# A chunked RWKV recurrence feeding a gated MLP: head pairs two levels apart instead of three, and the weights' low halves made by VectorE

## The chip, the cores and the metric

One Trainium2 chip, one core of it. The metric is device time in microseconds (us) of one execution, as the median of a few runs. Beside it stands one profiled execution, whose trace gives every instruction's start and duration. A core has TensorE (PE in the rows; its weight loads are PEld), VectorE (DVE), ScalarE (ACT), GpSimd (POOL) and SyncE (SP, which only issues DMAs here). The engines run their own instruction lists in order and meet through semaphores.

## What is computed

```python
def _attn_ref(r, k, v, w, u):                # r, k, v, w: [2, 8, 768, 48], u: [8, 48]
    for t in range(S):
        kt, vt, rt, wt = (k[:, :, t], v[:, :, t], r[:, :, t], w[:, :, t])
        cur = np.einsum('bhd,bhe->bhde', u[None] * kt, vt)
        y[:, :, t] = np.einsum('bhd,bhde->bhe', rt, state + cur)
        state = wt[:, :, :, None] * state + np.einsum('bhd,bhe->bhde', kt, vt)

x = y as [2, 768, 384]
h = gelu_tanh(x @ w_in)                      # w_in: [384, 1024]
u, v = h halves; v_n = layernorm(v) * g_ln
v_s = einsum('ts,bsd->btd', w_sg, v_n) + b_sg[None, :, None]
x2 = x + (u * v_s) @ w_out
xk, xr = mixes of x2 and x2 shifted by one token, by mu_k and mu_r
out = sigmoid(xr @ w_r) * (relu(xk @ w_k) ** 2 @ w_v)
```

## The kernel before

**The recurrence.** Two heads form a pair, 8 pairs q = 0 to 7 in all. The sequence of 768 is cut in 12 chunks of 64. Inside a chunk the score matrix with its decays is built in six levels: level 0 gives each token its own block and its partner's, level l joins blocks of 2^l tokens. For each level TensorE multiplies the scaled k by the scaled r (`level_job`, 12 x 2 matmuls), VectorE copies the wanted part into `aT` through a mask (`take_level`), and k and r are then scaled by products of w over blocks of that length: k by VectorE (`scale_k`, tile `kT`), r by VectorE up to level 2 (`scale_r`, tile `r2`) and by GpSimd from level 3 on. GpSimd also makes the products of w (`join`, tiles `wb`, `wchunk`). Level l can start only when both scalings of the level below are done.

**Jobs of a pair.** `w`, `k` and `r` are transposes of the loaded tokens (`turn_job`): TensorE into PSUM banks called `turn`, then ACT copies out (`copy_turn`), and VectorE makes the first scaled half of k and of r (`first_k`, `first_r`) straight from the same banks. The next transpose into these banks waits for both (`turn_free`). `kt` turns the scaled k back, ACT copies it to `ktok`; `u` multiplies it by v to the state increments; VectorE's `chain` scans them; `y` multiplies states and scores into the output, which ACT copies to `yT` and SP stores into `xT`, the transposed x. `sg` transposes one of six row blocks of w_sg, in the `turn` banks too.

**Slots.** The order of all engines comes from a table of slots. Pair q runs level l in slot 3q + l, so two pairs are under way, and there are 30 slots. `pair_jobs` places the other jobs, `SG_SLOTS` the w_sg transposes, `EARLY_DENSE` the first dense groups (the six V and eight U groups of batch 0, in slots 21 to 28), `joins` GpSimd's products.

**The dense part.** All dense matmuls are made exact to fp32 by halves: a = a_high + a_low, and three products of halves (`split`, three matmul lines). ACT casts the high halves of w_in, w_sg and w_out in 15 pieces, one a slot from slot 6 on (`SPLITS`); GpSimd subtracts to get the low halves two slots later (`low_half`). After the last slot TensorE runs the groups in the order G (w_sg), V, O, U, G, K, O, R, P, K, R, P. VectorE's `norm` and `apply_norm` make the layernorm of V of batch 0 in slots 24 and 25, with ACT's square root and casts `high_vn` between them; G needs the result, and w_sg's low halves.

**PSUM.** Eight banks: two `turn`, two for level jobs of even pairs and two of odd ones (`level`), two `ybanks`.

**Loads.** SP issues all DMAs in one list: pair loads wait for the r transpose two pairs back, loads of v for the y job four pairs back, stores of y for ACT's copy.

Of the kernel before, what the change touches and what calls it, by code (L numbers as in the profile page):

```python
# [15 lines left out]
def rwkv_gmlp_channel_mix_kernel(nc, r, k, v, w, u, w_in, g_ln, w_sg, b_sg, w_out,  # L16
# [25 lines left out]
    SLOTS = 3 * NP + LEVELS  # L42
# [7 lines left out]
    def pair_jobs(slot):  # L50

        a = slot // 3
        if slot % 3 == 0:
            jobs = [("kt", a - 2), ("w", a + 1), ("u", a - 2)]
        elif slot % 3 == 1:
            jobs = [("k", a + 1), ("y", a - 2)]
        else:
            jobs = [("r", a + 1)]
        return [(kind, q) for kind, q in jobs if 0 <= q < NP]

    def side_jobs(slot):


        jobs = [("sg", SG_SLOTS.index(slot))] if slot in SG_SLOTS else []
        return pair_jobs(slot) + jobs + EARLY_DENSE.get(slot, [])

    SG_SLOTS = [3, 4, 6, 7, 9, 10]
    EARLY_DENSE = {21: [("V", 0, 0), ("V", 0, 1)], 22: [("V", 0, 2), ("V", 0, 3)], 23: [("V", 0, 4), ("V", 0, 5)],
                   24: [("U", 0, 0), ("U", 0, 1)], 25: [("U", 0, 2), ("U", 0, 3)], 26: [("U", 0, 4), ("U", 0, 5)],
                   27: [("U", 0, 6)], 28: [("U", 0, 7)]}  # L70
# [10 lines left out]
    R_ZEROED, A_ZEROED, VT_ZEROED = (8, 10, 4, 5), (9, 11, 16, 17), 15  # L81
    K_SCALES = [(0, 0)]
    R_SCALES = [(0, 0)]
    for slot in range(SLOTS):
        if slot:
            K_SCALES += [(q, 0) for kind, q in pair_jobs(slot - 1) if kind == "k"]
            R_SCALES += [(q, 0) for kind, q in pair_jobs(slot - 1) if kind == "r"]
        K_SCALES += [(q, l) for q, l in level_jobs(slot) if l]
        R_SCALES += [(q, l) for q, l in level_jobs(slot) if 0 < l < DVE_R]
# [11 lines left out]
    def joins(slot):  # L101

        a, found = slot // 3, []
        for q, l in ([(a, 4), (a, 5), (a + 1, 0)], [(a + 1, 1), (a + 1, 2)], [(a + 1, 3)])[slot % 3]:
            if 0 < q < NP:
                found.append((q, l))
        return found
# [4 lines left out]
    def join_at(q, l):  # L112
        return JOINS.index((q, l)) + 1

    SPLITS = {6: ("in", 0), 7: ("in", 1), 8: ("in", 2), 9: ("in", 3), 10: ("in", 4), 11: ("in", 5),
              12: ("sg", 0), 13: ("sg", 1), 14: ("sg", 2), 15: ("sg", 3), 16: ("sg", 4), 17: ("sg", 5),
              18: ("out", 0), 19: ("out", 1), 20: ("out", 2)}
# [35 lines left out]
    with ExitStack() as ctx:  # L153
# [78 lines left out]
        kT, r2, aT, vt = [None] * 4, [None] * 4, [None] * 4, [None] * 4  # L232
# [9 lines left out]
        assert low[0] >= A_aT, (low[0], A_aT)  # L242
# [42 lines left out]
        level = [ps[:, 2:4, :], ps[:, 4:6, :]]  # L285
        ybanks = ps[:, 6:8, :]
        ybank = [ps[:, 6, :], ps[:, 7, :]]
# [116 lines left out]

        def turn_banks(job):
            kind, q = job
            if job == ("r", 0) or kind == "kt":
                return ybanks
            return level[1] if job == ("k", 0) else turn
# [14 lines left out]
        def _(sp):  # L424
# [76 lines left out]
        def _(pool):  # L501
# [36 lines left out]
            def scale_r(q, l):  # L538
# [6 lines left out]
                t = right2(r2[q % 4][0:ROWS, :, :], h)  # L545
# [3 lines left out]

            def low_half(slot):  # L550
                behind = slot - 2
                if behind in SPLITS:
                    lo, raw, hi = halves(SPLITS[behind])
                    pool.wait_ge(w_high, list(SPLITS).index(behind) + 1)
                    nc.gpsimd.tensor_tensor(lo, raw, hi.bitcast(F32), ALU.subtract).then_inc(w_low, 1)
# [24 lines left out]
            for s in (2, 3):  # L580
                nc.gpsimd.memset(r2[s][:, :, :], 0.0).then_inc(late_zeroed, 1)

            for slot in range(SLOTS):
                for q, l in joins(slot):
                    join(q, l)
# [3 lines left out]
                low_half(slot)  # L589
# [15 lines left out]
        def _(act):  # L605
            def copy_turn(job):
# [4 lines left out]
                if kind == "r":  # L611
                    if q < 4:
# [5 lines left out]
                    for x, (lo, hi) in enumerate(HEADS):  # L618
                        ins = nc.scalar.copy(by_parity(in_banks(r2[q % 4][lo:hi, x, :]))[:, 0],  # L619
# [131 lines left out]
            for slot in range(SLOTS):  # L751
# [14 lines left out]
                if slot == 18:  # L766
                    for m in range(MT):
                        high_x(0, m)
                if slot == 24:
                    root(0)  # L770
                if slot == 25:
# [39 lines left out]
        def _(dve):  # L811
# [20 lines left out]
            def first_r(q):  # L832
# [3 lines left out]
                for x, (lo, hi) in enumerate(HEADS):  # L836
                    ins = nc.vector.tensor_tensor(by_parity(in_banks(r2[q % 4][lo:hi, x, :]))[:, 1],
# [14 lines left out]
            def scale_r(q, l):  # L852
                h = 1 << l
                dve.wait_ge(r_scaled_dve, r_at(q, l - 1))
                t = right2(r2[q % 4][0:ROWS, :, :], h)
# [4 lines left out]
            def take_level(q, l):  # L860
                h = 1 << l
                dve.wait_ge(scores, level_at(q, l) + 1)
                if l == 0:
                    if q < 4:
                        dve.wait_ge(zeroed, A_ZEROED[q])
                    if q == 0:
# [4 lines left out]
                        level[q % 2][:, :, 0:HF].rearrange("p b (m t) -> p b m t", t=CH))  # L871
                else:
                    dve.wait_ge(masked, level_at(q, l - 1) + 1)
                    if q == 0:
# [5 lines left out]
                        level[q % 2][:, l % 2, 0:HF].rearrange("p (m n h) -> p m n h", m=2 * C, h=h))  # L880
                ins.then_inc(masked, 1)

            def chain(q):
# [6 lines left out]
                else:  # L890
# [8 lines left out]
                    in1=ybanks[0:ROWS, 1, 0:D], op0=ALU.mult, op1=ALU.add).then_inc(states, 1)  # L899

# [114 lines left out]
            for slot in range(SLOTS):  # L1015
                for kind, q in pair_jobs(slot - 1) if slot else []:
                    if kind == "k":
                        first_k(q)
                    elif kind == "r":
                        first_r(q)  # L1020
# [5 lines left out]
                for q, l in level_jobs(slot):  # L1026
# [4 lines left out]
                for kind, q in pair_jobs(slot):  # L1031
                    if kind == "u":
                        chain(q)
                if slot == 18:
                    for m in range(MT):
                        low_x(0, m)
                if slot == 19:
# [3 lines left out]
                if slot == 24:  # L1041
                    norm(0)
                if slot == 25:
# [23 lines left out]
        def _(pe):  # L1067
# [46 lines left out]
            def y_job(q):  # L1114
# [3 lines left out]
                for n in range(1, NCH):  # L1118
                    for x, (lo, hi) in enumerate(((0, 64), (64, ROWS))):
                        state = sc_last[0:ROWS, 0:hi - lo] if n == NCH - 1 else sc[0:ROWS, 0:hi - lo, n - 1]  # L1120
                        nc.tensor.matmul(ybanks[lo:hi, n % 2, n // 2 * CH:(n // 2 + 1) * CH], state,  # L1121
                                         r2[q % 4][0:ROWS, x, n * CH:(n + 1) * CH], start=(n < 3), stop=False,
# [9 lines left out]
            def level_job(q, l):  # L1132
                h = 1 << l
                if l == 0:
                    pe.wait_ge(copied, turn_at[("r", q)] + 1)
                    if q == 1:
                        pe.wait_ge(k_scaled, k_at(0, 0))
                    if q >= 2:
                        pe.wait_ge(masked, level_at(q - 2, LEVELS - 1) + 1)
                else:  # L1140
# [5 lines left out]
                    pe.wait_ge(masked, level_at(q, max(l - 2, 0)) + 1)  # L1146
                for c in range(C):
                    for g in range(2):
                        s = slice(c * P + g * CH, c * P + (g + 1) * CH)
                        if l == 0:  # L1150
                            ins = nc.tensor.matmul(  # L1151
                                level[q % 2][CHUNK[g], c // 3, c % 3 * P:(c % 3 + 1) * P].rearrange("p (x t) -> p x t", x=2),
                                kU[0:ROWS, s], rU[0:ROWS, :, s], start=True, stop=True)
                        else:
                            ins = nc.tensor.matmul(  # L1155
                                level[q % 2][CHUNK[g], l % 2, c * CH:(c + 1) * CH].rearrange("p (x t) -> p x t", x=2),
                                kT[q % 4][0:ROWS, s], right2(r2[q % 4][0:ROWS, :, s], h), start=True, stop=True)
# [79 lines left out]
            for slot in range(SLOTS):  # L1237
                for q, l in level_jobs(slot):
                    level_job(q, l)
# [40 lines left out]
```

## Time and profile before

| what | us |
| --- | --- |
| median of 3 runs | 449.48 |
| lowest and highest | 448.78, 451.25 |
| the profiled execution, device time | 453.91 |
| its span, first to last instruction | 452.2 |
| TensorE busy | 390.1 |
| VectorE busy | 259.6 |
| ScalarE busy | 182.5 |
| GpSimd busy | 145.1 |

The span is what the trace shows. The profiled execution took 1.7 us more than its span and 4.4 us more than the median. Times inside the trace are counted from the span's start. A row of a timeline gives start, duration, engine, line and operation, what it writes and reads, how many instructions were merged, and in brackets how long the engine had stood idle and what released it; "issue" there means that the profile names no releaser.

### The profile page before, as it was taken

The numbers are of one execution on the slowest core, as the hardware profiler recorded it, in microseconds if no ns is written. First come the engines' busy times: TensorE is split into PE (matmuls) and PEld (weight loads), VectorE is DVE, ScalarE is ACT, GpSimd is POOL, SyncE is SP. The second block draws the span as 40 slices with busy tenths as digits, with TensorE's granted clock in tenths as the row PEclk, the third lists the DMA queues.
The fourth block names the chain that finished last, engine by engine and source line by source line (L and its number), as shares of the span: only waits on it lengthen the run. The fifth ranks groups of instructions, "written<-read, shape, count | busy, mean of one in ns | idle before, by whom it ended". The sixth has DMA issues, their size and how long they took to land.

```text
span 452.2 us, 9083 instructions
## 1 busy us (share of the span) xinstructions
PE 390.1 (86%) x3836; PEld 367.9 (81%) x3836; DVE 259.6 (57%) x369; ACT 182.5 (40%) x318; POOL 145.1 (32%) x153
## 2 busy tenths in 40 slices
PE   3767687867676679988699999999999999999997
PEld 2656577757666568877599989999999999999997
DVE  6735575768596972667326543599879601565001
ACT  4332554454455233245332140662686630265100
POOL 7624253748393931331000000052195000084000
PEclk9955896988798857999599999999999999999999
DMA  8996423241420100101010000030500001100011
GB/s 157 255 268 194 80 57 77 48 87 39 95 55 2 28 1 1 28 2 28 1 28 1 1 0 1 0 141 0 191 4 1 0 19 52 36 0 1 0 54 52
DMA packets 58584, 23.59 MB, mean 52 GB/s; under 512 B 52656, under 2 KB 56112, under 8 KB 58544
## 3 DMA queue, kind: packets, MB, share of 16 engines
q1 hardware_dynamic: 58544, 23.02, 20.2%
q8 instruction: 30, 0.49, 0.5%
q14 instruction: 10, 0.08, 0.1%
HBM read 18.29 MB, written 2.36 MB: 46 GB/s over the span
## 4 chain that ended last, share of the span: by engine, by line
PE 79%; issue 8%; DVE 7%; ACT 4%; DMA 1%; SPq 1%; ACTq 0%; DVEq 0%
PE ps L1164 18%; PE ps L1165 18%; PE ps L1166 18%; PE ps L1155 7%; PE ps L1151 5%; DVE kT L849 4%; PE ps L1121 3%; PE ps L1088 3%; PE ps L1110 3%; PE ps L1093 2%; PE ps L1098 1%; ACT ktok L641 1%; PE ps L1126 1%; ACT r L619 1%; DVE vn_l L942 1%
## 5 line engine op out<-in xcount | busy, mean ns | idle before, releaser
L1155 PE MATMUL ps<-r,kT 112*64 112x64 f32 x960 | 40.8, 249 | 29.4 <-issue 21.7
L1155 PEld LDWEIGHTS ps<-r,kT 112*64 112x64 f32 x960 | 37.0, 161 | 35.2 <-issue 25.9
L849 DVE TENSOR_TENSOR kT<-kT,wb 112x384 f32<-112x384 f32 x40 | 41.0, 1032 | 30.5 <-PE ps L1155 29.2
L601 POOL TENSOR_TENSOR sq_f<-sq_f 128x384 f32<-128x384 f32 x32 | 33.7, 1071 | 74.9 <-ACT sq_f L734 74.8
L546 POOL TENSOR_TENSOR r<-r,wb 112x768 f32<-112x768 f32 x24 | 39.9, 1663 | 50.8 <-PE ps L1155 50.8
L1010 DVE TENSOR_TENSOR ot<-ps,ee 128x384 f32<-128x384 f32 x12 | 6.7, 558 | 54.6 <-PE ps L1166 54.6
L995 DVE TENSOR_TENSOR sq_l<-sq_f,sq_h 128x384 fp32r<-128x384 f32 x32 | 27.7, 864 | 10.3 <-ACT sq_h L739 10.3
L1166 PE MATMUL ps<-xk_h,wk_l 128*128 128x384 f32 x96 | 32.2, 335 | 0.0
L1165 PE MATMUL ps<-xk_l,wk_h 128*128 128x384 f32 x96 | 32.2, 335 | 0.0
L1164 PE MATMUL ps<-xk_h,wk_h 128*128 128x384 f32 x96 | 32.2, 335 | 0.0
L1164 PE MATMUL ps<-wv_h,sq_h 128*128 128x384 f32 x96 | 32.1, 334 | 0.0
L1166 PE MATMUL ps<-wv_h,sq_l 128*128 128x384 f32 x96 | 32.1, 334 | 0.0
L1165 PE MATMUL ps<-wv_l,sq_h 128*128 128x384 f32 x96 | 32.1, 334 | 0.0
L1164 PE MATMUL ps<-wsg_h,vn_h 128*128 128x384 f32 x96 | 32.1, 334 | 0.0
L1165 PE MATMUL ps<-wsg_l,vn_h 128*128 128x384 f32 x96 | 32.1, 334 | 0.0
L1166 PE MATMUL ps<-wsg_h,vn_l 128*128 128x384 f32 x96 | 32.1, 334 | 0.0
L596 POOL TENSOR_TENSOR wk_l<-wk_raw,wk_h 128x1024 fp32r<-128x1024 f32 x3 | 8.2, 2778 | 65.1 <-ACT wk_h L797 65.1
L1151 PE MATMUL ps<-rU,kU 112*64 112x128 f32 x192 | 22.4, 421 | 7.2 <-ACT r L619 7.2
L1151 PEld LDWEIGHTS ps<-rU,kU 112*64 112x64 f32 x192 | 19.8, 228 | 8.0 <-ACT r L619 8.0
L893 DVE TENSOR_TENSOR_SCAN sc<-wm,ps 112x480 f32<-112x480 f32 x8 | 9.2, 1154 | 27.4 <-PE ps L1110 27.4
L876 DVE COPY_PREDICATED aT<-mask,ps 128x384 f32<-128x384 int8 x40 | 24.8, 656 | 0.2
L856 DVE TENSOR_TENSOR r<-r,wb 112x768 f32<-112x768 f32 x16 | 24.9, 1558 | 0.0
(150 smaller groups left out, 994.6 us busy)
## 6 DMA issues: line engine op xcount, KB each, us to landing
tok_w<-in_w_dram SPq DMA_DIRECT2D x16, 144.0 KB, 3.0
tok_k<-in_k_dram SPq DMA_DIRECT2D x16, 144.0 KB, 3.3
tok_r<-in_r_dram SPq DMA_DIRECT2D x16, 144.0 KB, 3.1
vt<-in_v_dram SPq DMA_DIRECT2D x16, 144.0 KB, 3.3
sgn<-in_moe_w_sg_dram SPq DMA_DIRECT2D x6, 384.0 KB, 5.1
out_dram<-ot SPq DMA_DIRECT2D x12, 192.0 KB, 1.9
xT<-yT SPq DMA_DIRECT2D x12, 144.0 KB, 2.7
win_raw<-in_moe_w_in_dram SPq DMA_DIRECT2D x1, 1536.0 KB, 9.1
```

The costliest lines, as they stand in the source:

```text
L546: nc.gpsimd.tensor_tensor(t, t, pair_of(h, 0, q).unsqueeze(1).unsqueeze(3).broadcast_to([ROWS, 2, S // (2 * h), h]), ALU.mult).then_inc(r_ ...
L601: nc.gpsimd.tensor_tensor(t, t, t, ALU.mult).then_inc(k_sq, 1)
L849: nc.vector.tensor_tensor(t, t, pair_of(h, 1, q).unsqueeze(2).broadcast_to([ROWS, S // (2 * h), h]), ALU.mult).then_inc(k_scaled, 1)
L856: nc.vector.tensor_tensor(t, t, pair_of(h, 0, q).unsqueeze(1).unsqueeze(3).broadcast_to([ROWS, 2, S // (2 * h), h]), ALU.mult).then_inc(r_ ...
L876: ins = nc.vector.copy_predicated(right(aT[q % 4][:, :, :, :].rearrange("p c x t -> p (c x t)"), h), mask[:, l - 1, 0:CH // 2].unsqueeze(1 ...
L995: nc.vector.tensor_tensor(sq_l[:, f, c], sq_f[:, f, c], sq_h[:, f, c].bitcast(F32), ALU.subtract).then_inc(k_low, 1)
L1088: ins = nc.tensor.transpose(dst[0:ROWS, c // 3, c % 3 * P:(c % 3 + 1) * P], tok[q % 2][kind][:, c, :], ident[:, :])
L1151: ins = nc.tensor.matmul(level[q % 2][CHUNK[g], c // 3, c % 3 * P:(c % 3 + 1) * P].rearrange("p (x t) -> p x t", x=2), kU[0:ROWS, s], rU[0 ...
L1155: ins = nc.tensor.matmul(level[q % 2][CHUNK[g], l % 2, c * CH:(c + 1) * CH].rearrange("p (x t) -> p x t", x=2), kT[q % 4][0:ROWS, s], righ ...
L1164: nc.tensor.matmul(acc, ah, bh, start=(i == 0), stop=False)
L1165: nc.tensor.matmul(acc, ah, bl, start=False, stop=False)
L1166: ins = nc.tensor.matmul(acc, al, bh, start=False, stop=(i == n - 1))
```

## The change

Pairs now run two levels apart: pair q has level l in slot 2q + l, three pairs are under way, and there are 22 slots. One table, `pe_jobs`, now gives TensorE's order with the levels placed between the other jobs; ACT follows its side jobs. The two banks of level 0 and 1 are shared by all pairs (`young`), levels 2 and 3 have one bank (`middle`), levels 4 and 5 another (`old`). There is a fifth `r2` buffer. VectorE takes each level right behind its scalings, pair by pair, and makes the 15 low halves, in slots 3 to 8 (w_in), 14 to 19 (w_sg) and 20, 20, 21 (w_out). ACT's casts of the high halves start in slot 2. GpSimd scales r ahead of its joins. The w_sg transposes go to slots 3, 5, 7, 9, 11 and 13, the V groups to slots 16 to 18, the U groups to 19 to 21. SP loads w_in ahead of pair 3, spreads the w_sg loads, asks for pairs earlier, and loads the bias after the last store of y.

```diff
-    SLOTS = 3 * NP + LEVELS
+    SLOTS = 2 * NP + LEVELS
...
-        return [(q, slot - 3 * q) for q in (slot // 3 - 1, slot // 3) if 0 <= q < NP and 0 <= slot - 3 * q < LEVELS]
+        return [(q, slot - 2 * q) for q in (slot // 2 - 2, slot // 2 - 1, slot // 2)
+                if 0 <= q < NP and 0 <= slot - 2 * q < LEVELS]
...
+    def pe_jobs(slot):
+
+        a = slot // 2
+        if slot % 2 == 0:
+            jobs = [("kt", a - 3), ("level", a - 2, 4), ("level", a - 1, 2), ("w", a + 1), ("level", a, 0), ("u", a - 3),
+                    ("k", a + 1)]
         else:
-            jobs = [("r", a + 1)]
-        return [(kind, q) for kind, q in jobs if 0 <= q < NP]
+            jobs = [("level", a - 2, 5), ("level", a - 1, 3), ("r", a + 1), ("level", a, 1), ("y", a - 3)]
+        jobs = [job for job in jobs if 0 <= job[1] < NP]
+        jobs += [("sg", SG_SLOTS.index(slot))] if slot in SG_SLOTS else []
+        return jobs + EARLY_DENSE.get(slot, [])
...
-    SG_SLOTS = [3, 4, 6, 7, 9, 10]
+    SG_SLOTS = [3, 5, 7, 9, 11, 13]
+    EARLY_DENSE = {16: [("V", 0, 0), ("V", 0, 1)], 17: [("V", 0, 2), ("V", 0, 3)], 18: [("V", 0, 4), ("V", 0, 5)],
+                   19: [("U", 0, 0), ("U", 0, 1), ("U", 0, 2)], 20: [("U", 0, 3), ("U", 0, 4), ("U", 0, 5)],
+                   21: [("U", 0, 6), ("U", 0, 7)]}
...
+        return [(q, slot - 2 * q + 1) for q in range(1, NP) if 0 <= slot - 2 * q + 1 < LEVELS]
...
+    SPLITS = {2: ("in", 0), 3: ("in", 1), 4: ("in", 2), 5: ("in", 3), 6: ("in", 4), 7: ("in", 5),
+              8: ("sg", 0), 9: ("sg", 1), 10: ("sg", 2), 11: ("sg", 3), 12: ("sg", 4), 13: ("sg", 5),
+              14: ("out", 0), 15: ("out", 1), 16: ("out", 2)}
+    LOW_SLOTS = [3, 4, 5, 6, 7, 8, 14, 15, 16, 17, 18, 19, 20, 20, 21]
...
-        level = [ps[:, 2:4, :], ps[:, 4:6, :]]
+        young, middle, old = ps[:, 2:4, :], ps[:, 4, :], ps[:, 5, :]
...
             load_pair(2)
+            sp.dma_start(win_raw[:, :, :], w_in.rearrange("(m p) f -> p m f", p=P)).then_inc(win_in, 16)
+            load_pair(3)
+            load_sg(0)
+            load_sg(1)
             load_v(0)
-            for t in range(C):
+            load_pair(4)
+            for t in range(2, C):
                 load_sg(t)
             load_v(1)
-            load_pair(3)
-            sp.dma_start(win_raw[:, :, :], w_in.rearrange("(m p) f -> p m f", p=P)).then_inc(win_in, 16)
+            load_pair(5)
...
-            sp.dma_start(bbc[:, :], b_sg.rearrange("(a s) -> a s", a=1).broadcast_to([P, S])).then_inc(bias_in, 16)
             for q in range(NP):
-                if q + 4 < NP:
-                    load_pair(q + 4)
                 store_y(q)
                 if q + 4 < NP:
                     load_v(q + 4)
+                if q + 6 < NP:
+                    load_pair(q + 6)
+            sp.wait_ge(turned, turn_at[("r", 6)] + 1)
+            sp.dma_start(bbc[:, :], b_sg.rearrange("(a s) -> a s", a=1).broadcast_to([P, S])).then_inc(bias_in, 16)
...
             for slot in range(SLOTS):
-                for q, l in joins(slot):
-                    join(q, l)
                 for q, l in level_jobs(slot):
                     if l >= DVE_R:
                         scale_r(q, l)
-                low_half(slot)
+                for q, l in joins(slot):
+                    join(q, l)
...
                     if 0 < l < DVE_R:
                         scale_r(q, l)
-                for q, l in level_jobs(slot):
                     take_level(q, l)
...
+                for n in range(PIECES):
+                    if LOW_SLOTS[n] == slot:
+                        low_half(n)
...
-                    if q == 1:
-                        pe.wait_ge(k_scaled, k_at(0, 0))
-                    if q >= 2:
-                        pe.wait_ge(masked, level_at(q - 2, LEVELS - 1) + 1)
+                    if q:
+                        pe.wait_ge(masked, level_at(q - 1, 1) + 1)
...
-                    pe.wait_ge(masked, level_at(q, max(l - 2, 0)) + 1)
+                    if l % 2:
+                        pe.wait_ge(masked, level_at(q, l - 1) + 1)
+                    elif q:
+                        pe.wait_ge(masked, level_at(q - 1, l + 1) + 1)
```

What this makes of the order is shown at two places. In these lists `ident` with a `tok` tile is a token transpose, with `kT` the kt job, with `sgn` a w_sg transpose; `rU,kU` is a level 0, `r2...,kT...` a later level, `vt,ktok` the u job (44 matmuls, left out behind the first), `sc` the beginning of a y job.

TensorE, around the period of one pair in the steady part, before:

```order
L1098 MATMUL ps<-ident_58,sgn_79 128x128 x6
L1155 MATMUL ps<-r22_93,kT2_94 64x64 x12
L1155 MATMUL ps<-r23_89,kT3_90 64x64 x12
L1088 MATMUL ps<-ident_58,tok_r0_110 112x128 x6
L1155 MATMUL ps<-r23_89,kT3_90 64x64 x12
L1151 MATMUL ps<-rU_105,kU_104 64x128 x12
L1093 MATMUL ps<-ident_58,kT2_94 128x112 x6
L1088 MATMUL ps<-ident_58,tok_w1_108 112x128 x6
L1110 MATMUL ps<-vt2_91,ktok_83 64x48
```

TensorE, from one w_sg transpose to the y job of the next slot, after:

```order
L1104 MATMUL ps<-ident_58,sgn_79 128x128 x6
L1099 MATMUL ps<-ident_58,kT2_95 128x112 x6
L1162 MATMUL ps<-r23_90,kT3_91 64x64 x12
L1162 MATMUL ps<-r24_87,kT0_103 64x64 x12
L1094 MATMUL ps<-ident_58,tok_w0_112 112x128 x6
L1158 MATMUL ps<-rU_106,kU_105 64x128 x12
L1116 MATMUL ps<-vt2_92,ktok_83 64x48
...
L1094 MATMUL ps<-ident_58,tok_k0_110 112x128 x6
L1162 MATMUL ps<-r23_90,kT3_91 64x64 x12
L1162 MATMUL ps<-r24_87,kT0_103 64x64 x12
L1094 MATMUL ps<-ident_58,tok_r0_111 112x128 x6
L1162 MATMUL ps<-r20_102,kT1_99 64x64 x12
L1127 MATMUL ps<-r22_94,sc_80 64x64
```

The kt job and the u job had one transpose between them and now have two levels, a transpose and a level 0; the w_sg transpose now follows a y job and stands ahead of kt and of both levels of the next slot.

VectorE, one odd slot and what follows it, before (levels of two pairs, scalings of both ahead of the copies):

```order
L828 TENSOR_TENSOR kT0_102<-ps,wT_103 112x384
L849 TENSOR_TENSOR kT2_94<-kT2_94,wb0_84 112x12x32
L849 TENSOR_TENSOR kT3_90<-kT3_90,wb1_85 112x96x4
L856 TENSOR_TENSOR r23_89<-r23_89,wb1_85 112x192x4
L876 COPY_PREDICATED aT2_92<-mask_76,ps 128x12x32
L876 COPY_PREDICATED aT3_88<-mask_76,ps 128x96x4
L837 TENSOR_TENSOR r20_101<-ps,wT_103 48x384 x2
```

VectorE, odd slot 7 and the head of slot 8, after:

```order
L827 TENSOR_TENSOR kT0_103<-ps,wT_104 112x384
L848 TENSOR_TENSOR kT1_99<-kT1_99,wb1_85 112x12x32
L875 COPY_PREDICATED aT1_97<-mask_76,ps 128x12x32
L848 TENSOR_TENSOR kT2_95<-kT2_95,wb0_84 112x48x8
L875 COPY_PREDICATED aT2_93<-mask_76,ps 128x48x8
L848 TENSOR_TENSOR kT3_91<-kT3_91,wb1_85 112x192x2
L855 TENSOR_TENSOR r23_90<-r23_90,wb1_85 112x384x2
L875 COPY_PREDICATED aT3_89<-mask_76,ps 128x192x2
L903 TENSOR_TENSOR win_l_50<-win_raw_51,win_h_49 128x512
L836 TENSOR_TENSOR r24_87<-ps,wT_104 48x384 x2
```

Between first k and the next first r there were five operations and are now eight, the last of them a low half.

## Rows read from the trace of the kernel before

**Rows 1.** The page: the span, and the clock granted to TensorE by slice.

```profile
span 452.2 us, 9083 instructions
...
PEclk9955896988798857999599999999999999999999
```

**Rows 2.** One steady stretch: length, each engine's busy time, granted clock, DMA share, GB/s.

```profile
115.00:138.00 23.00, 16.44 (x321) 15.11 (x319) 17.25 (x20) 10.23 (x17) 14.51 (x12) 0.87 0.28 57
```

**Rows 3.** The chain that ended last: start, duration, what (L1151 is level 0).

```profile
12.17 2.83 PE ps L1151 x24
...
41.02 2.76 PE ps L1155 x48
...
48.10 2.83 PE ps L1151 x24
...
164.81 2.83 PE ps L1151 x24
...
178.02 1.55 PE ps L1155 x48
179.57 2.47 PE ps L1121 x35
...
193.90 0.74 PE ps L1093 x6
...
196.15 1.48 PE ps L1110 x42
```

**Rows 4.** TensorE's timeline: two waits, the V and U groups' edges, the first G group.

```profile
101.47 1.82 PE L1155 MATMUL ps<-r,kT 112*64 112x64 f32 x48 [1.81 <-issue]
...
114.21 1.55 PE L1155 MATMUL ps<-r,kT 112*64 112x64 f32 x24 [3.64 <-DVE kT L849]
...
182.82 0.50 PE L1164 MATMUL ps<-win_h,x_h 128*128 128x512 f32 x1
...
187.13 1.62 PE L1155 MATMUL ps<-r,kT 112*64 112x64 f32 x48
...
205.04 0.44 PE L1164 MATMUL ps<-x_h,win_h 128*128 128x384 f32 x1
...
208.37 0.92 PE L1155 MATMUL ps<-r,kT 112*64 112x64 f32 x24
...
217.05 1.35 PE L1093 MATMUL ps<-ident,kT 112*128 112x112 f32 x6 [4.44 <-DVE kT L849]
...
230.76 0.33 PE L1164 MATMUL ps<-wsg_h,vn_h 128*128 128x384 f32 x1
```

**Rows 5.** VectorE's timeline: one duration for each kind of its operations.

```profile
92.87 1.12 DVE L837 TENSOR_TENSOR r<-ps,wT 48x384 f32<-48x384 f32 x2
...
95.97 1.03 DVE L868 COPY_PREDICATED aT<-mask_first,ps 128x768 f32<-128x768 int8 x1 [0.80 <-PE ps L1151]
99.72 1.15 DVE L893 TENSOR_TENSOR_SCAN sc<-wm,ps 112x480 f32<-112x480 f32 x1 [2.73 <-PE ps L1110]
...
103.81 2.58 DVE L856 TENSOR_TENSOR r<-r,wb 112x768 f32<-112x768 f32 x1
...
113.13 0.97 DVE L856 TENSOR_TENSOR r<-r,wb 112x768 f32<-112x768 f32 x1
114.03 1.02 DVE L876 COPY_PREDICATED aT<-mask,ps 128x384 f32<-128x384 int8 x2
...
211.81 0.68 DVE L942 TENSOR_TENSOR vn_l<-vv,vn_h 128x512 fp32r<-128x512 f32 x1
```

**Rows 6.** GpSimd's timeline: the first join of a pair, and a scaling of r.

```profile
99.03 0.83 POOL L528 TENSOR_TENSOR wb<-wT 112x384 f32<-112x384 f32 x1 [6.66 <-ACT wT L634]
...
104.06 1.52 POOL L546 TENSOR_TENSOR r<-r,wb 112x768 f32<-112x768 f32 x1
```

**Rows 7.** Line L849 from 90 to 160: count, ns shortest/median/longest, first and last start.

```profile
L849 DVE TENSOR_TENSOR kT<-kT,wb x14: 559/996/3839, 88.4 to 152.5; 112x384 f32<-112x384 f32 x14
```

**Rows 8.** ACT's groups by line, 0 to 230: shapes, count, busy us, mean ns, idle before.

```profile
L627 ACT ACTIVATE kU<-ps,ucol 112x384 f32<-112x384 f32 x8 | 5.0, 625 | 0.0
```

More of the change, by code:

```diff
@@ L85, in rwkv_gmlp_channel_mix_kernel @@
         if slot:
-            K_SCALES += [(q, 0) for kind, q in pair_jobs(slot - 1) if kind == "k"]
-            R_SCALES += [(q, 0) for kind, q in pair_jobs(slot - 1) if kind == "r"]
+            K_SCALES += [(job[1], 0) for job in side_jobs(slot - 1) if job[0] == "k"]
+            R_SCALES += [(job[1], 0) for job in side_jobs(slot - 1) if job[0] == "r"]
         K_SCALES += [(q, l) for q, l in level_jobs(slot) if l]
@@ L408, in turn_banks @@
                 return ybanks
-            return level[1] if job == ("k", 0) else turn
+            return first_k_banks if job == ("k", 0) else turn
         def last_turn(job):
@@ L548, in scale_r @@
                     ALU.mult).then_inc(r_scaled_pool, 1)
[L550 to L555, printed above, removed]
             def later_masks():
@@ L899, in chain, with low_half @@
                     in1=ybanks[0:ROWS, 1, 0:D], op0=ALU.mult, op1=ALU.add).then_inc(states, 1)
+            def low_half(n):
+                lo, raw, hi = halves(list(SPLITS.values())[n])
+                dve.wait_ge(w_high, n + 1)
+                nc.vector.tensor_tensor(lo, raw, hi.bitcast(F32), ALU.subtract).then_inc(w_low, 1)
             def low_x(b, m):
@@ L1015, in _ @@
             for slot in range(SLOTS):
[L1016 to L1020, printed above, removed]
+                for job in side_jobs(slot - 1) if slot else []:
+                    if job[0] == "k":
+                        first_k(job[1])
+                    elif job[0] == "r":
+                        first_r(job[1])
                 for q, l in level_jobs(slot):
@@ L1030, in _ @@
                         nc.vector.memset(aT[s][:, :, :, :], 0.0).then_inc(zeroed, 1)
[L1031 to L1034, printed above, removed]
+                for job in side_jobs(slot):
+                    if job[0] == "u":
+                        chain(job[1])
+                for n in range(PIECES):
+                    if LOW_SLOTS[n] == slot:
+                        low_half(n)
+                if slot == 15:
                     for m in range(MT):
                         low_x(0, m)
-                if slot == 19:
+                if slot == 16:
                     dve.wait_ge(params_in, 48)
@@ L1155, in level_job @@
                             ins = nc.tensor.matmul(
[L1156 to L1157 removed]
+                                level_bank(l)[CHUNK[g], c * CH:(c + 1) * CH].rearrange("p (x t) -> p x t", x=2),
+                                kT[q % 4][0:ROWS, s], right2(r2[q % 5][0:ROWS, :, s], h), start=True, stop=True)
                 ins.then_inc(scores, 1)
@@ L1237, in _ @@
             for slot in range(SLOTS):
-                for q, l in level_jobs(slot):
-                    level_job(q, l)
-                for job in side_jobs(slot):
-                    if job[0] == "y":
+                for job in pe_jobs(slot):
+                    if job[0] == "level":
+                        level_job(job[1], job[2])
+                    elif job[0] == "y":
                         y_job(job[1])
```

60 lines of the change are left out of this document (23 added, 37 removed).

## The prediction, made before the changed kernel was run

> **What bounds the kernel now.** I read the slices first, then the stretches, then the chain that ended last, then each engine's timeline. The span falls into two stages. From 230.76 on TensorE runs the dense groups without a gap at the full clock; before that it is busy in 5 to 9 tenths of a slice and the clock dips [rows 1, 4]. The last stage is bound by matmuls that the change leaves alone, so the question is when the group at 230.76 can start. In the stage ahead, TensorE is busy 16.4 of 23 us with a granted clock of 0.87, VectorE 17.3, GpSimd 14.5 [rows 2]: no engine is full, and waits decide. The level-0 jobs of pairs 2 and 7 start at 48.10 and 164.81 [rows 3]: 116.7 us for five pairs, **23.3 us a pair**. Two gaps show why. At 101.47 TensorE had stood still for 1.81 us: GpSimd did its join (99.03, itself held back by ACT) ahead of the scaling that the level needs. At 114.21 it had stood still for 3.64 us behind VectorE's scaling of kT [rows 4, 6], an operation that takes 0.56 us at its shortest and 3.84 at its longest [rows 7]. The first is a question of order, the second of VectorE and GpSimd standing in each other's way: the 768-wide scaling takes VectorE 0.97 us alone and 2.58 us when it starts at 103.81 beside GpSimd's operation of 104.06 [rows 5, 6].
>
> The Trainium skill, "SBUF — State Buffer", section "SBUF: two separate sides", says of this that the port pair shared by VectorE and GpSimd is an exclusive lock held for the whole instruction. The trace agrees where it shows 2.58 for 0.97. By that rule a low half moved to VectorE still shuts GpSimd out; what that would cost is the first rival below.
>
> **Work of one pair, which the change keeps.** TensorE: five levels of 0.78 (1.55 for two), level 0 at 2.8, the transpose of kT 0.74 and three token transposes taken as the same (0.8), the increments 1.5, the y job from 179.57 to 182.82 = 3.3 [rows 3, 4]. Sum 3.9 + 2.8 + 0.7 + 2.4 + 1.5 + 3.3 = **14.6 us**, 15.4 with a w_sg transpose. At the lower clock level two levels took 2.76 instead of 1.55 [rows 3]. VectorE alone: six kT operations at 0.56, two r scalings at 0.97, first r 1.12, five level copies at 0.51, the first at 1.03, scan and last state 1.5 [rows 5, 7]: 3.4 + 1.9 + 1.1 + 2.6 + 1.0 + 1.5 = **11.5 us**. GpSimd: three scalings at 1.5 [rows 6], and joins: between 0.83 (one row) and 4 (the 14.5 us of rows 2 less three scalings and three low halves of about 2); the sizes halve from join to join, so I take 2.7. Sum 7.2.
>
> **Part 1, the low halves.** Fifteen subtractions leave GpSimd, 1.3 to 2 us each there by what rows 2 leave over, and come to VectorE at 0.68 for 512 columns [rows 5], about 0.9 for 768. VectorE's load rises to about 12.1 us a pair (six pieces in slots 3 to 8, none in 9 to 13, the rest in 14 to 21), GpSimd's falls by 4 us a pair. This takes the longest blocker out of VectorE's way. In even slots a piece lies before a wait and costs nothing; in odd slots it delays the first r scaling, 0.7 us.
>
> **Part 2, two slots a pair.** I walk one pair's period, time 0 at the kt job of an even slot, all at full clock. TensorE: kt 0.7, L4 1.5, L2 2.3, w 3.1, L0 5.9, u 7.4, k 8.2. The copy of kt is now hidden behind L4, L2, w and L0. ACT's three copies of k, about 0.6 each [rows 8], end at 9.8 and VectorE's first k at 10.3. Meanwhile L5 and L3 run (to 9.7), and r, which needs the same banks, runs to 11.1, L1 to 11.9, y to 15.2. VectorE in the odd slot has seven operations after 10.3, 4.0 us alone; GpSimd's two scalings fall between them, which I take at 1.6 us of delay (nothing at best, 3.0 if it waits for both in full): 15.9. Its first r of the next pair then ends at 17.0. **Here stands the new wait**: in slots 3, 5, ..., 13 the w_sg transpose is the last job of the odd slot, writes the banks that r used, and so waits for that first r. TensorE stands still from 15.2 to 17.0, then transposes to 17.8, and queued behind it are kt, L4 and L2, for which VectorE in turn waits. A period is 17.8 us, 18.5 where a low half is in the odd slot. VectorE in the even slot (levels from 1.6, first copy at 5.9 or later, chain after u at 7.4) ends near 9.5 and holds nobody up. The lower clock costs more: of TensorE's jobs some 5 us lie on this path and double. At 0.87 granted, a quarter of the time is at the lower level, +1.3. I take **19.2 us a pair**, bounds 16.3 (TensorE alone, 15.4 and handovers) and 22.2.
>
> **The start.** L0 of pair 0 stays at 12.2 [rows 3]. The r transpose of pair 1 now stands ahead of L1 of pair 0 and waits for k's copies and first k, so L0 of pair 1 comes near 25, no gain. The next period is at the lower clock, as before: r and sg wait one after the other, 19 us, to 44 (48.10 before). The one after has no y job: 17 us, to 61. Four periods at 19.2 give **L0 of pair 7 at 138** (164.81 before). The loads are asked for a pair or more earlier, and w_in's weights come ahead of pair 3. I cost this at nothing: the first needs of pair 3 are at slot 4, some 20 us after its issue. If the DMAs were late, up to 5 us.
>
> **The tail.** From L0 of pair 7 to the first G group it was 66.0 us. The V and U groups have fewer slots, and more attention is left: two V groups take 4.3 (182.82 to 187.13), two U groups 3.3 (205.04 to 208.37) [rows 4]. After: L0 and u 4.0, L5, L3, L1 and y 5.7, slot 16 about 10 (V waits for x_low, which waits for y's copy and ACT's casts), slot 17 9, slot 18 8: the last V group ends 37 us after L0. From there on L5, y and three U groups take TensorE to +9; it then waits, as it did for 4.44 us at 217.05 [rows 4], for the norm of V, since ACT copies kt of pair 7 only behind the six casts of vn: to about +17. Then u, three U, y, two U: +30, and some 4 more at the lower clock that such a wait brought at 217 (1.35 us for that kt, 0.74 at full clock [rows 3, 4]). 37 + 34 = **71 us**, 5 more than before. Moving the bias load behind the last store costs nothing: the first gate would come some us later at most, and TensorE has eight banks of G groups to fill before it needs that bank back.
>
> **Sum.** 138 + 71 = 209 against 230.8: 21.8 us less. Span 452.2 - 21.8 = 430.4, the profiled execution (453.9) becomes 432.1; the median of the runs is 449.5, so I put **427.7**.
>
> **Rivals.**
> 1. *The two engines exclude each other in full.* VectorE's 12.1 + GpSimd's 7.2 + 2.4 in which VectorE waits for L4 behind the w_sg transpose + clock 0.5 = 22.2 a pair: 61 + 89 + 71 = 221, 10 us gained, **440**. For it: 3.84 against 0.56 [rows 7]. Against: level copies and PSUM reads, half of VectorE's work, keep their time beside GpSimd. By the rule of the skill cited above this would be the case for each scaling. Chance 0.18.
> 2. *TensorE becomes the bound.* 16.3 a pair, full clock, tail 67: 61 + 65 + 67 = 193, 38 us gained, **412**. For it: three pairs give TensorE something to do in most waits. Against: the w_sg wait. Chance 0.12.
> 3. *It doesn't do what it says*: three pairs in one fixed order lock the engines into steps, rival 1 plus another 1.6 for ACT's copies of k = 23.8, no shorter than before: 61 + 95 + 71 = 227, **446** or a little more. Chance 0.06.
> 4. *The clock stays at its lower level from slot 6 on*, because small waits are now spread evenly. TensorE's period is then 23.1 + 2.7 = 25.8, the tail +25: 61 + 103 + 96 = 260, **479**, slower. It decides from a share of about 0.57 at the lower level (22 us of the 51 that lie between my quarter and the whole). For it: the granted clock dips to 5 to 8 tenths in slices of this stage [rows 1]. Against: TensorE's idle share falls from 0.28 to about 0.2. Chance 0.07.
>
> **Numbers.** Forecast 0.57 (418 to 434), rivals as given. About 0.5% is what a measurement of this kernel can tell from no change. Faster 0.87, same 0.06, slower 0.07. Range 413 to 444.
>
> **What would show it.** L0 of pairs 2, 3 and 7 near 44, 61 and 138, with 18 to 20 us between them from pair 3 on; a gap ahead of each w_sg transpose of about 2 us that ends with first r; kT operations that are seldom over 2 us; ACT's kt copy no longer waited for; the first G group near 209, after a gap of 7 us ahead of the last u job; 221 to 222 us from there to the end. If L0 of pair 7 is past 150, the periods are wrong; if the distance to G is over 76, the tail is.

## The result

The changed kernel took 424.55 us (median of 4 runs, 420.25 to 427.84) against 449.13 us before: a ratio of 0.942, 95% interval 0.933 to 0.951. Run again beside the experiments it took 422.34 against 451.01: 0.939, 0.931 to 0.947. The forecast was 427.7, range 413 to 444, faster.

The page after, to be read against [rows 1]: the span, TensorE's busy tenths, the clock granted.

```profile
span 422.7 us, 9085 instructions
...
PE   5576496979879699939999999999999999999997
...
PEclk9776878889997999969999999999999999999999
```

The first G group starts at 201.33 instead of 230.76 [rows 4]; from there to the end it is 221.4 us in both, to a tenth. So the whole difference lies ahead of it. The stretch up to the first G group, before and then after (length, TensorE, weight loads, VectorE, ScalarE, GpSimd busy with counts, granted clock, DMA share, GB/s):

```profile
0.00:230.76 230.76, 171.70 (x2594) 151.93 (x2595) 144.45 (x198) 96.25 (x162) 102.99 (x116) 0.83 0.32 74
```

```profile
0.00:201.33 201.33, 154.70 (x2594) 139.71 (x2595) 140.19 (x213) 96.06 (x162) 81.86 (x102) 0.88 0.37 84
```

TensorE runs the same 2594 matmuls in both. It is idle for 230.76 - 171.70 = 59.1 us before and 46.6 after, 12.4 less; and it is **busy for 17.0 us less with the same work**. In these two traces the larger part of the 29.4 us is not waits removed but instructions that became shorter, as the granted clock rose from 0.83 to 0.88. The traces overstate it: the spans differ by 29.5 us and the medians by 24.6, since the profiled execution of before was 4.4 us above its median and that of after at its own. Executions of the kernel before went from 442.85 us at a granted clock of 0.950 over the span to this one, 453.91 at 0.913. If all of the 4.9 us between the two differences lies in the clock, 12.1 of 24.6 us are shorter instructions, about half; that is an estimate.

Levels 0 of pairs 3, 4, 5 and 7 in TensorE's timeline of after, which answer to [rows 3]:

```profile
58.73 1.53 PE L1158 MATMUL ps<-rU,kU 112*64 112x128 f32 x24
...
78.58 1.53 PE L1158 MATMUL ps<-rU,kU 112*64 112x128 f32 x24
...
96.81 1.53 PE L1158 MATMUL ps<-rU,kU 112*64 112x128 f32 x24
...
131.17 2.10 PE L1158 MATMUL ps<-rU,kU 112*64 112x128 f32 x24
```

From pair 3 to pair 7 it is 72.4 us, 18.1 a pair, where it was 23.3. A level 0 takes 1.53 us where the rows of before had 2.83 at 48.10 and 164.81. All of them together, before and after:

```profile
L1151 PE MATMUL ps<-rU,kU 112*64 112x128 f32 x192 | 22.4, 421 | 7.2 <-ACT r L619 7.2
```

```profile
L1158 PE MATMUL ps<-rU,kU 112*64 112x128 f32 x192 | 14.4, 307 | 2.2 <-ACT r L618 2.2
```

That is 8.0 of the 17.0 us. Before, each level 0 stood right behind a wait or one level job behind a longer one (3.64 us at 114.21 [rows 4]), and all eight took 2.68 to 2.83 us, the lower clock level. Now most of them stand behind three or four jobs in a row, and five of the eight (pairs 2 to 6) take 1.53.

The predicted new wait, around slot 11: TensorE's rows, then VectorE's.

```profile
106.61 0.92 PE L1132 MATMUL ps<-aT,vt 64*64 64x64 f32 x48
109.54 0.84 PE L1104 MATMUL ps<-ident,sgn 128*128 128x128 f32 x6 [2.00 <-issue]
```

```profile
107.48 0.99 DVE L875 COPY_PREDICATED aT<-mask,ps 128x384 f32<-128x384 int8 x1
108.27 1.16 DVE L836 TENSOR_TENSOR r<-ps,wT 48x384 f32<-48x384 f32 x2
111.85 0.56 DVE L848 TENSOR_TENSOR kT<-kT,wb 112x384 f32<-112x384 f32 x1 [2.42 <-PE ps L1162]
```

The w_sg transpose starts at 109.54, when first r has ended at 109.43, and VectorE then stands still for 2.42 us until L4 is done behind it. Ahead of the six transposes TensorE stands still for 4.04, 5.89, 3.03, 2.25, 2.00 and 2.01 us. In the tail:

```profile
178.93 0.74 PE L1099 MATMUL ps<-ident,kT 112*128 112x112 f32 x6
186.61 2.58 PE L1116 MATMUL ps<-vt,ktok 128*64 128x48 f32 x44 [6.94 <-ACT ktok L640]
```

6.94 us ahead of the last u job, and the clock falls behind it: 2.58 us for a u job, where the one at 196.15 before took 1.48 [rows 3]. (The last u job of before took 2.58 as well, at 219.93, behind its own waits of 4.44 and 1.53 us.)

### The profile page after: what moved, and what is told of

Read it like the earlier page. It is cut to its first block, busy times and chain, and to the rows that moved or that the text cites. A ratio compares the mean times of both kernels' runs of the same rounds, so it can differ in the third digit from the quotient of the medians.

```text
span 422.7 us, 9085 instructions
## 1 busy us (share of the span) xinstructions
PE 373.2 (88%) x3836; PEld 355.7 (84%) x3836; DVE 255.4 (60%) x384; ACT 182.3 (43%) x318; POOL 124.0 (29%) x139
## 3 DMA queue, kind: packets, MB, share of 16 engines
q1 hardware_dynamic: 58544, 23.02, 21.8%
## 4 chain that ended last, share of the span: by engine, by line
PE 83%; issue 7%; DVE 4%; ACT 3%; DMA 1%; SPq 1%; DVEq 0%; ACTq 0%
PE ps L1171 19%; PE ps L1172 19%; PE ps L1173 19%; PE ps L1162 7%; PE ps L1094 5%; PE ps L1127 4%; PE ps L1158 3%; PE ps L1116 2%; PE ps L1104 2%; PE ps L1132 1%; PE ps L1099 1%; ACT rU L615 1%; ACT r L618 1%; DVE kT L848 1%; DVE r L855 1%
## 5 line engine op out<-in xcount | busy, mean ns | idle before, releaser
L553 POOL TENSOR_TENSOR r<-r,wb 112x768 f32<-112x768 f32 x24 | 42.7, 1791 | 86.1 <-PE ps L1162 86.1
L848 DVE TENSOR_TENSOR kT<-kT,wb 112x384 f32<-112x384 f32 x40 | 38.5, 964 | 30.7 <-PE ps L1162 30.3
L1162 PEld LDWEIGHTS ps<-r,kT 112*64 112x64 f32 x960 | 35.3, 157 | 6.6 <-issue 3.7
L1162 PE MATMUL ps<-r,kT 112*64 112x64 f32 x960 | 39.0, 245 | 1.6 <-DVE r L855 1.6
L875 DVE COPY_PREDICATED aT<-mask,ps 128x384 f32<-128x384 int8 x40 | 26.5, 662 | 0.2
L1104 PE MATMUL ps<-ident,sgn 128*128 128x128 f32 x36 | 8.4, 401 | 19.2 <-issue 19.2
L1104 PEld LDWEIGHTS ps<-ident,sgn 128*128 128x128 f32 x36 | 6.3, 208 | 19.9 <-issue 19.9
L710 ACT CAST g_h<-uT 128x384 fp32r<-128x384 f32 x16 | 8.2, 514 | 33.9 <-DVE uT L966 33.9
L1116 PE MATMUL ps<-vt,ktok 128*64 128x48 f32 (+1 forms) x352 | 12.7, 229 | 9.3 <-ACT ktok L640 9.3
```

The costliest lines, as they stand in the source:

```text
L553: nc.gpsimd.tensor_tensor(t, t, pair_of(h, 0, q).unsqueeze(1).unsqueeze(3).broadcast_to([ROWS, 2, S // (2 * h), h]), ALU.mult).then_inc(r_ ...
L848: nc.vector.tensor_tensor(t, t, pair_of(h, 1, q).unsqueeze(2).broadcast_to([ROWS, S // (2 * h), h]), ALU.mult).then_inc(k_scaled, 1)
L875: ins = nc.vector.copy_predicated(right(aT[q % 4][:, :, :, :].rearrange("p c x t -> p (c x t)"), h), mask[:, l - 1, 0:CH // 2].unsqueeze(1 ...
L1104: ins = nc.tensor.transpose(dst[:, j // 3, (j % 3) * P:(j % 3 + 1) * P], sgn[:, q, j * P:(j + 1) * P], ident[:, :])
L1116: ins = nc.tensor.matmul(to, ktok[:, n % 2, n // 2, lo:hi], vt[q % 4][:, n // 2, lo:lo + D], start=True, stop=True)
L1162: ins = nc.tensor.matmul(level_bank(l)[CHUNK[g], c * CH:(c + 1) * CH].rearrange("p (x t) -> p x t", x=2), kT[q % 4][0:ROWS, s], right2(r2[ ...
```

## The experiments

All ran three rounds beside the kernel before (the last one five); times are medians. "Changed" is the changed kernel run again on the chip of the first four, 422.3 us. Experiments 5 to 8 ran on a second chip and 9 to 11 on a third, where the kernel before took 450.85 and 449.01 us instead of 451.01; against "changed" the ratios to before are then the safer comparison.

**1. The changed kernel again.** 

> The changed kernel once more, as the yardstick on the chip of the next three. Both theories expect 0.94 of the time before (423 to 425 us).

Measured: 422.34, ratio 0.939. It is the yardstick. In its trace pair 7's level 0 is at 130.66 and the first G group at 200.62, within 0.8 us of the first trace.

**2. The low halves back on GpSimd.**

```diff
-                dve.wait_ge(w_high, n + 1)
-                nc.vector.tensor_tensor(lo, raw, hi.bitcast(F32), ALU.subtract).then_inc(w_low, 1)
+                pool.wait_ge(w_high, n + 1)
+                nc.gpsimd.tensor_tensor(lo, raw, hi.bitcast(F32), ALU.subtract).then_inc(w_low, 1)
```

> The changed kernel with the 15 low halves given back to GpSimd, in the same slots, behind its scalings and joins. Theory (the low halves on GpSimd block VectorE, which the path runs through in odd slots, for 1.3 to 2 us each): 4 to 9 us slower than the changed kernel, a larger gap ahead of the w_sg transposes of slots 3, 5 and 7, and the last V group later. Rival (the slot spacing carries the gain, a low half at the end of GpSimd's slot lies in its idle time): within 2 us of the changed kernel.

Measured: 431.28, ratio 0.959 (0.953 to 0.965), 9 us slower than changed. The size is the theory's, the place mostly not. The gaps ahead of the w_sg transposes of slots 3, 5 and 7 are 4.48, 6.35 and 3.08 us instead of 4.03, 5.87 and 3.01, and pair 3's level 0 is at 60.69 instead of 59.19. By pair 7 only 0.5 us of that is left (131.13 against 130.66). A good part came back behind the gap of slot 7, where TensorE's jobs happened to run at the full clock (5.2 us from the w_sg transpose to level 0 instead of 6.1), so the steady part costs 0.5 to 1.5 us. The rest falls in the tail, 77.2 us from pair 7's level 0 to the first G group (at 208.35) instead of 70.0. TensorE shows where:

```profile
150.33 0.47 PE L1171 MATMUL ps<-win_h,x_h 128*128 128x512 f32 x1 [2.12 <-DVE x_l L910]
...
183.01 0.44 PE L1171 MATMUL ps<-x_h,win_h 128*128 128x384 f32 x1 [2.17 <-ACT uT L699]
```

The first V group starts 19.2 us behind level 0 instead of 15.5: GpSimd, with its low halves between the scalings, meets two kT operations of VectorE (2.40 and 2.18 us, 0.57 and 0.54 in changed) and then x_l, whose three subtractions take 5.21 us in this kernel and 2.69 in changed. The first two V groups behind these waits run in part at the lower clock, 5.9 us instead of 4.3. That is 5.3 of the 7.3 us. The U group at 183.01 loses another 1.8 us (its wait was 0.38 in changed): ACT comes late with uT, since its square root ahead of that waits 4.98 us for VectorE in the norm. Here is VectorE there, then GpSimd:

```profile
175.29 4.80 DVE L926 TENSOR_SCALAR lnve<-lnmv 128x6 f32<-128x6 f32 x1
```

```profile
174.29 1.50 POOL L553 TENSOR_TENSOR r<-r,wb 112x768 f32<-112x768 f32 x1 [3.45 <-PE ps L1162]
175.75 1.82 POOL L560 TENSOR_TENSOR wsg_l<-wsg_f,wsg_h 128x768 fp32r<-128x768 f32 x1
177.52 3.78 POOL L560 TENSOR_TENSOR wout_l<-wout_raw,wout_h 128x512 fp32r<-128x512 f32 x3
```

An addition on six elements a partition took 4.80 us, while GpSimd had five operations one behind the other. With the low halves on VectorE the same addition takes:

```profile
169.87 0.21 DVE L923 TENSOR_SCALAR lnve<-lnmv 128x6 f32<-128x6 f32 x1
```

Of these 4.6 us TensorE had covered all but 1.8 with other groups.

**3. GpSimd's joins ahead of its scalings.**

```diff
-                for q, l in level_jobs(slot):
-                    if l >= DVE_R:
-                        scale_r(q, l)
                 for q, l in joins(slot):
                     join(q, l)
+                for q, l in level_jobs(slot):
+                    if l >= DVE_R:
+                        scale_r(q, l)
```

> The changed kernel with GpSimd's joins ahead of its scalings of r in each slot, as before the change. Theory (with one whole slot between a scaling and the level that needs it, the order on GpSimd has slack: a scaling ends near 104.6 and its level starts at 110.9): 0 to 2 us slower than the changed kernel. Rival (the order was what ended the 1.8 us wait of before): 5 us slower or more, a wait ahead of L4 or L5.

Measured: 421.12, ratio 0.935 (0.931 to 0.940): no difference to changed that could be told. With a whole slot of slack the order on GpSimd is free.

**4. The w_sg transpose behind level 0.**

```diff
-    SG_SLOTS = [3, 5, 7, 9, 11, 13]
+    SG_SLOTS = [4, 6, 8, 10, 12, 14]
...
-        jobs += [("sg", SG_SLOTS.index(slot))] if slot in SG_SLOTS else []
+        if slot in SG_SLOTS:
+            jobs.insert(jobs.index(("level", a, 0)) + 1, ("sg", SG_SLOTS.index(slot)))
```

The later casts (`SPLITS`, one slot each) are left out here.

> The changed kernel with the w_sg transpose placed behind level 0 in slots 4, 6, ..., 14 instead of at the end of slots 3, 5, ..., 13; ACT's casts of w_sg and w_out come one slot later. Theory (the w_sg transpose behind the r transpose makes kt, L4 and L2 wait for VectorE's first r: gaps of 4.0, 5.9, 3.0, 2.3, 2.0 and 2.0 us, and VectorE waits for L4 in turn): the gaps go or halve, 8 to 14 us faster than the changed kernel, level 0 of pair 7 near 120. Rival (VectorE and GpSimd together are the bound, the gap only moves to the w transpose): 0 to 4 us faster.

Measured: 416.28, ratio 0.925 (0.919 to 0.930), 6.1 us faster than changed: between the two. Pair 7's level 0 is at 120.02, as the theory had it. From pair 4 on TensorE's gaps are down to 0.6 us at the r transpose and the wait for the copy of y:

```profile
117.85 0.79 PE L1100 MATMUL ps<-ident,kT 112*128 112x112 f32 x6 [0.93 <-ACT yT L664]
118.57 1.62 PE L1163 MATMUL ps<-r,kT 112*64 112x64 f32 x48
120.02 1.48 PE L1159 MATMUL ps<-rU,kU 112*64 112x128 f32 x24
```

But from there to the first G group (192.87) it is 72.9 us instead of 70.0. The last w_sg transpose now lies in that part (0.8 us), and a u job and the first two V groups ran in part at the lower clock, 2.5 and 6.1 us instead of 1.5 and 4.3. 10.6 - 2.9 = 7.7 us are left in the trace. The sum had counted the gain up to a point and not what came behind it.

**5. The norm one slot later.**

```diff
-                if slot == 19:
+                if slot == 20:
                     for j in range(C):
                         high_vn(0, j)
...
-                if slot == 19:
+                if slot == 20:
                     apply_norm(0)
```

> The changed kernel with VectorE's apply_norm and ACT's six casts of vn for batch 0 in slot 20 instead of 19, behind the copy of kt of pair 7, the chain and three gelus. Theory (TensorE's 6.9 us wait ahead of the last u job is ACT's copy of kt queued behind the casts): the wait falls under 2 us, the clock doesn't fall behind it, 5 to 9 us faster than the changed kernel. Rival (the first G group then waits for vn_low instead): 0 to 3 us faster, a new wait ahead of the first G group.

Measured: 415.82, ratio 0.924 (0.917 to 0.930), 6.5 us faster than changed. The wait ahead of the last u job falls from 6.94 to

```profile
179.87 1.48 PE L1116 MATMUL ps<-vt,ktok 128*64 128x48 f32 x44 [1.53 <-ACT ktok L640]
```

and the job itself from 2.58 to 1.48. The first G group starts at 193.40; the rival's wait for vn_low is there, but only 0.33 us long.

**6. Both of these.** 

> Both edits: the w_sg transpose behind level 0 and the norm one slot later. Theory: the two gaps lie one behind the other and add up, 13 to 22 us faster than the changed kernel. Rival (each lets the other's wait grow): under 10 us faster.

Measured: 408.89, ratio 0.910 (0.903 to 0.917), 13.4 us faster than changed. They add up: 6.1 + 6.5 = 12.6.

**7. The kernel before, low halves on VectorE.**

```diff
-                    pool.wait_ge(w_high, list(SPLITS).index(behind) + 1)
-                    nc.gpsimd.tensor_tensor(lo, raw, hi.bitcast(F32), ALU.subtract).then_inc(w_low, 1)
+                    dve.wait_ge(w_high, list(SPLITS).index(behind) + 1)
+                    nc.vector.tensor_tensor(lo, raw, hi.bitcast(F32), ALU.subtract).then_inc(w_low, 1)
```

> The kernel before with the low halves made by VectorE at the end of the same slots, nothing else. Theory (a low half on GpSimd costs VectorE more wait than its own 0.7 to 0.9 us): 5 to 12 us faster than before, level 0 of pair 7 from 164.8 to near 156. Rival (VectorE was the busier engine already and only gets more): 0 to 5 us slower than before.

Measured: 440.54 against 450.85, ratio 0.979 (0.973 to 0.984), 10.3 us faster than before. In the traces pair 7's level 0 moves from 164.81 to 150.66. VectorE's kT operations in this part (shortest, median and longest in ns, then the first and last start), before and then here:

```profile
L849 DVE TENSOR_TENSOR kT<-kT,wb x27: 544/593/3839, 42.6 to 160.5; 112x384 f32<-112x384 f32 x27
```

```profile
L841 DVE TENSOR_TENSOR kT<-kT,wb x28: 542/560/1799, 40.4 to 164.8; 112x384 f32<-112x384 f32 x28
```

VectorE has more to do and the kernel is faster.

**8. The same, and GpSimd's scalings ahead of its joins** (the edit of 3 the other way round, in the kernel before). 

> The kernel before with the low halves made by VectorE and GpSimd's scalings ahead of its joins, still three slots a pair. Theory (two causes of wait go, the levels' round trips stay): 10 to 17 us faster than before, so that about half of the change's 26 us is the two slots a pair. Rival (the spacing carries it): at most 5 us faster.

Measured: 433.13, ratio 0.963 (0.957 to 0.968), 17.7 us faster than before, a shade beyond the expected 10 to 17. At three slots a pair the order that was free in 3 is worth 7.4 us. From here to the changed kernel it is 10.8 us, less than half of the whole: that is what two slots a pair bring over a kernel that has the other two parts, together with the new order of jobs, banks, casts and loads. No run takes these apart.

**9. The kernel before, its gaps filled with idle work.**

```diff
+            def fill(bank, n):
+                for _ in range(n):
+                    nc.tensor.transpose(bank[:, 0:P], ident[:, :], ident[:, :])
...
+                if 6 <= slot < 22 and slot % 3 == 0:
+                    pe.wait_ge(masked, level_at(slot // 3 - 2, 4) + 1)
+                    fill(level[slot // 3 % 2][:, 0, :], 16)
+                if 6 <= slot < 22 and slot % 3 == 1:
+                    pe.wait_ge(masked, level_at(slot // 3 - 1, 2) + 1)
+                    fill(level[(slot // 3 - 1) % 2][:, 0, :], 7)
```

> The kernel before with idle work for TensorE in its two gaps a pair: 16 transposes of the identity (2.1 us at full clock) ahead of the levels of slots 6, 9, ..., 21 and 7 (0.9 us) ahead of those of slots 7, 10, ..., 19, into a free bank whose content nobody reads. Theory (more than half of the change's gain, 17.0 of 29.4 us in the traces, is that the same TensorE instructions run at the full clock, because it is not left idle): 6 to 12 us faster than before although work is added, level 0 at 1.4 instead of 2.6 to 2.8 us. Rival (the waits set the end, a faster level is waited for all the same): within 2 us of before.

Measured: 440.88 against 449.01, ratio 0.986 (0.980 to 0.992), so 8.1 us faster by the medians and 6.4 by the ratio. Work was added, no wait was taken out of the program, and the kernel is faster. The stretch up to its first G group, and the fill in it:

```profile
0.00:217.19 217.19, 170.45 (x2726) 152.62 (x2726) 144.93 (x198) 96.41 (x162) 103.27 (x116) 0.93 0.34 78
```

```profile
L1104 PE MATMUL ps<-ident 128*128 128x128 f32 x131 | 17.8, 291 | 0.0
```

The granted clock is 0.93 instead of 0.83. Of the 170.45 us busy 17.8 are fill, so the kernel's own matmuls take 152.7 us instead of 171.7. The rival (the waits take it back) explains only a part: 19.0 us shorter, 13.6 of them reach the first G group. Both are against the trace of before at 453.91; by the medians it is 8.1. Level 0 is at the full clock in five of the eight pairs, and not in all.

**10. The changed kernel, its w_sg gaps filled.** The same `fill` into the bank of levels 4 and 5, once VectorE has read level 5, ahead of each w_sg transpose. 

> The changed kernel with such transposes ahead of each w_sg transpose, 24, 30, 18, 12, 12 and 12 of them for its gaps of 4.0, 5.9, 3.0, 2.3, 2.0 and 2.0 us. Theory (the clock): granted clock up to the first G group from 0.88 to above 0.92, 3 to 7 us faster than the changed kernel. Rival (waits): 0 to 1 us, or slower by what the fill overshoots its gap.

Measured: 417.14, ratio 0.932 (0.926 to 0.939), 5.2 us faster than changed by the medians and 2.9 by the ratios, whose intervals overlap (0.926 to 0.939 here, 0.931 to 0.947 there). In the trace the clock is at 0.95 up to the first G group, the kernel's own matmuls take 145.9 us (158.97 busy less 13.1 of fill) instead of 154.9, and the group starts at 193.26 instead of 200.62. So the clock had more to give; how much of it reaches the kernel's time, these runs don't settle.

**11. Experiment 6 with the joins first.** 

> The w_sg transpose behind level 0, the norm one slot later, and GpSimd's joins ahead of its scalings (which was 1 us faster by itself, within the noise). Either theory: within 2 us of 408.9.

Measured: 407.04, ratio 0.911 (0.906 to 0.917) in five rounds. It can't be told from 6. These two are the fastest here, 42 us below the kernel before in the median, 0.09 in the ratio.

## Why the prediction was right, step by step

- **What bounds.** Right. The dense part kept its 221.4 us, and everything came from the stage ahead of it.
- **The start.** Levels 0 of pairs 1, 2 and 3 were put at 25, 44 and 61, and stood at 24.87, 41.01 and 58.73. The late r transpose is there, with 2.23 us of wait for k's copies. The loads cost nothing: behind 7 us the profile puts no wait of TensorE down to a DMA. The period up to pair 2 was put at the lower clock, 19 us, and took 16.1, with k, r and two levels at the full one from 27.17 to 31.95.
- **The period.** 19.2 us were forecast and 18.1 measured, so pair 7's level 0 was put at 138 and came at 131.2. The structure was right: the wait at the w_sg transpose (2 us, ended by first r), the wait of 0.6 us at the r transpose, kt's copy hidden. **The term that failed is level 0 at 2.8 us.** I put it down as a time at full clock, and it was one at the lower level, as all eight levels 0 of before were; at the full one it takes 1.53. I had asked what the lower clock costs the jobs that I thought quick, and not whether the durations that I started from were quick ones. With 1.3 us less the period is 17.9. The walk shows the same: first r was to end 17.0 us behind kt, and behind the kt at 110.22 it ended 15.7 later. The four periods were 19.9, 18.2, 16.4 and 17.9; only their mean is near the forecast's constant one.
- **The clock.** I took 0.87 granted for the steady part and it was 0.87 between pair 2's and pair 7's level 0. But I set that against before's 0.87, read from a stretch of 23 us; over the same pairs it was 0.84 before, and 0.83 against 0.88 over the whole stage. The forecast thus held nothing for the clock, where the traces show 17.0 us of shorter matmuls, 8.0 of them in level 0. These are one error and not two: a level 0 priced at 2.8 is a gain from the clock left out.
- **Part 1, the low halves.** Right in sign and mostly wrong in place; the sum gave them no size of their own. I had put their use in the steady part's VectorE; experiment 2 shows 0.5 to 1.5 us there and 7 us in the tail. In the kernel before they did cost the steady part (experiment 7, 14 us in the trace at pair 7). Their own price was as forecast: the w_sg gap is 3.03 us in slot 7, with a low half ahead of it, and 2.0 to 2.25 in slots 9 to 13 without one. In slot 7 of experiment 2 the r scaling takes 2.02 instead of 0.95 us, but VectorE is spared its own low half of 0.72, and TensorE's gap there is 3.08 instead of 3.01 us: in that slot the two prices nearly cancel.
- **The tail.** 71 us forecast, 70.2 measured, the wait of the last u job 7 and 6.94, and the lower clock behind it as expected. Experiment 5 settles its cause.
- **The rivals.** Full exclusion (440) didn't come: kT's operations stay under 2 us. They do meet GpSimd more often than I thought: between 40 and 163 their median is 1120 ns, where it was 593 before. TensorE as the bound (412) didn't either, but experiment 6 comes below its number once the waits at the w_sg transpose and the last u job are gone: 15.7 us a pair from pair 3 on, with TensorE busy for 56.7 of 62.8 us at a granted clock of 0.98. The clock at its lower level throughout (479) had the mechanism right and its sign wrong: the clock is what a denser order gains.
- **The sum.** 209 for the first G group against 201.3, 6.8 of it at pair 7's level 0 (2.3 from the start, the rest from the period) and 0.8 from the tail. So the trace moved by 29.5 us where 21.8 were forecast, 7.7 off. By the medians it is 24.6, and the forecast of 427.7 is only 3.2 us off. That is luck: the trace that I worked from was an execution 4.4 us slower than the median, and this took up more than half of the error.

## What to carry to other kernels

Before a duration goes into a sum, see at which clock level it was taken: here every level 0 of the kernel before stood close behind a wait of TensorE, and no row of it showed the full clock's price. Count TensorE's busy time for the same instructions before and after, beside its idle time; where it falls, the order has bought clock, and a few idle matmuls in a gap test in one run whether there is more to buy. When two engines get in each other's way, look at which jobs meet there rather than at which engine is busier: VectorE was the busier one, and taking over 15 operations from GpSimd made both kernels faster.

## What was not expected of the hardware

A tiny VectorE operation can wait through several GpSimd operations in a row: 4.80 us for six elements, until about the end of the fourth of GpSimd's five (experiment 2; the last three stand merged in one row, which I divide by three). The kernel before had it already: the 2.58 us at 103.81 [rows 5] began beside the joins of the row below and ended at 106.39, 0.8 us behind the GpSimd scaling of 104.06 [rows 6], which had started later than it.

```profile
102.55 1.55 POOL L528 TENSOR_TENSOR wb<-wb 112x192 f32<-112x192 f32 x2
```

The other way round, a GpSimd scaling of 1.5 us took 5.06 while VectorE ran operations without a pause, in the changed kernel run again:

```profile
142.43 5.06 POOL L553 TENSOR_TENSOR r<-r,wb 112x768 f32<-112x768 f32 x1 [3.67 <-PE ps L1162]
```

The Trainium skill ("SBUF — State Buffer", "SBUF: two separate sides") has the loser block for the winner's whole instruction; here the block lasts longer. If the scaling's own 1.5 us are the last of its 5.06, it was kept out until about 146.0, through the end of a low half, three x_l subtractions and a kT operation, so a run of operations on one side has to be counted whole.

Idle work can pay: 131 transposes of the identity, 17.8 us of TensorE's time, made the kernel before 8.1 us faster by the medians (experiment 9).
